# Attention in a fused kernel: the product with v streams the probabilities past the v of two heads, and a second product turns it back

## The chip, the core and the metric

The kernel runs on one core of one Trainium2 chip. The metric is device time in microseconds, of which lower is better. TensorE does matrix products (PE in the profile; the loads of its stationary operand are listed as PEld), VectorE is DVE, ScalarE ACT, GpSimd POOL, and SyncE (SP) starts most transfers.

## The reference

Attention for 4 batches of 8 heads of 576 rows, 64 wide, in which a query sees itself and the 127 keys before it; its output feeds two mixture layers, of which only the first part matters here: the gate of the first mixture takes the logits from the attention output.

```python
B, H, S, D = q.shape                                   # 4, 8, 576, 64
scores = scale * np.matmul(q, k.transpose(0, 1, 3, 2))
bias = slopes[:, None, None] * (-np.abs(rel))[None]
mask = (rel >= 0) & (rel < 128)
scores = np.where(mask, scores + bias[None], -1e9)
attn = softmax(scores)                                 # over keys
x = np.matmul(attn, v)                                 # -> (B * S, H * D) = (2304, 512)
logits = x @ w_gate                                    # 512 x 8; each row goes to the expert of its largest logit
# first mixture: x by expert, relu(x @ w1[e]) @ w2[e]; second mixture: 4 dense experts, mixed by domain_probs
```

## The kernel before

Everything is float32 or the pair of float32r values (high and low part) that stand for one. The first 190 us or so are attention; after that come the sparse mixture and, over the last two thirds, the dense one, which the change does not touch.

**Tiling.** A head has QT = 5 query tiles of 128, 128, 128, 128 and 64 rows. Tile 0 sees one block of 128 keys, the others two (the last one 128 and 64). A pair is two heads, and there are NP = 16 pairs, four a batch. A step is one tile of one head, and a duo is two steps, so that there are 80 duos, five for each pair. Steps are counted through a head before the next one, so that the five duos of a pair are tiles (0,1), (2,3), (4,0), (1,2), (3,4).

**Order.** Each engine runs one loop over duo numbers, written out in the program. TensorE in round j does `scores(j)` (L1570, L1571: q times the high and the low part of k, two float32r products a step), one tile of `gate_v` (L1613), `turn_probs(j-2)` (L1582, transposes of the probabilities against an identity), and `pv(j-4)` (L1599). VectorE adds mask and position bias and takes the maximum (`mask_scores`, L1144), ScalarE exponentiates (`soften`, L862) and copies the transposed probabilities out of PSUM (`copy_turned`, L870).

**The product with v.** `pv` has the turned probabilities stationary (128 keys x 128 queries) and streams v of one head. v has 73 useful columns a head: 64 of v, a column of ones whose product is the softmax denominator, and 8 columns v x w_gate, which `gate_v` computes ahead from a transposed copy of v (`v_turned`, loaded by SyncE) and ScalarE copies into place (`copy_vg`, L876). The stream is made 102 columns wide (PV_N), that of `gate_v` 86 (VG_N). A float32 product is listed as two passes, each with its load of the stationary operand. When a head's five tiles are done, VectorE takes denominators, reciprocals and two products out of PSUM (`norm_sum`, `norm_inverse`, `norm`; L1156, L1160, L1165, L1167), once a head.

**What else the rounds carry.** While pair n runs, the q and k of pair n+1 are split: VectorE casts (`split_hi`, L1106, two in each of the first two rounds of a pair) and GpSimd subtracts (`split_qk`, L569 and L577). TensorE's `scores` waits for it at the pair's start (`qk_lo`). When a batch's last head is done, its routing runs on VectorE a step a round: `batch_due(j, after)` says in which round, counted from round 20 + PV_LAG of the batch. Step 8 is `add_ranks` (L1270), step 9 `put`, after which GpSimd scatters the rows of x to their experts (`scatter`, L618). GpSimd's own order is fixed: for batch 0 the scatter stands between `split_qk(7)` and `split_qk(8)`, and for batch 1 the choice of the first experts (`chosen`, step 15, L1298), weight loads and a scatter stand ahead of `split_qk(13)`. After the loop GpSimd scatters batch 2, upon which SyncE loads the first rows (L494) and TensorE turns them in round 82 (`turn_rows(0)`, L1631), ahead of the `pv` of the last duo.

## Time and profile before

| | us |
|---|---|
| median of 3 runs | 1217.76 (1215.81 to 1221.4) |
| the profiled execution's own time | 1216.41 |
| its span, first to last instruction | 1214.8 |
| TensorE busy in the span | 1192.8 (98%) |
| VectorE, ScalarE, GpSimd busy | 726.4, 420.0, 794.2 |
| mean granted TensorE clock | 0.996 |
| loads of v with ones; of v turned | 16 x 365.0 KB; 16 x 288.0 KB |

Busy is the union of an engine's instructions; a TensorE product's listed duration is longer than the distance to the next one, because products overlap. What a product costs in a stream is therefore read from the distance between starts. A granted clock of 1.00 is 2.4 GHz, and 0.50 is 1.2 GHz.

### The profile page before, as it was taken

How to read it: one execution, taken by the hardware profiler on the slowest of the kernel's cores; microseconds unless marked ns; L12 is line 12 of the kernel's file. 1: busy time of each engine (PE TensorE's matmuls, PEld its weight loads, DVE VectorE, ACT ScalarE, POOL GpSimd, SP SyncE). 2: the span in 40 equal slices, each digit the busy share in tenths (PEclk: the TensorE clock that was granted, in tenths of full speed). 3: DMA queues.
4: the chain of work that ended last, by engine and by line, in shares of the span. 5: the costliest groups of instructions: out<-in, count | busy, mean ns of one | idle time of the engine just before them, and what ended most of it. 6: DMA issues, size and time to landing. Idle time of an engine off the chain costs nothing.

```text
span 1214.8 us, 18910 instructions
## 1 busy us (share of the span) xinstructions
PE 1192.8 (98%) x6446; PEld 1051.0 (87%) x6447; DVE 726.4 (60%) x1600; ACT 420.0 (35%) x766; POOL 794.2 (65%) x527
## 2 busy tenths in 40 slices
PE   8999999999999999999999999999999999999997
PEld 6888887788888888999889999999999999899996
DVE  7876987232222247666666666666666666666664
ACT  5655552111111143333333333333333333333330
POOL 5465685856666766658758776678578676666652
PEclk9998999999999999999999999999999999999999
DMA  7855687988888703212111132121211221111101
GB/s 280 278 199 175 244 310 242 338 308 320 320 319 320 304 27 123 79 53 77 70 70 70 70 122 96 70 87 62 86 70 70 81 92 60 66 68 70 70 35 52
DMA packets 46635, 177.79 MB, mean 146 GB/s; under 512 B 9312, under 2 KB 15584, under 8 KB 30176
## 3 DMA queue, kind: packets, MB, share of 16 engines
q1 hardware_dynamic: 29680, 121.57, 28.0%
q0 software_dynamic: 7520, 43.07, 9.6%
q10 hardware_dynamic: 9360, 12.17, 3.0%
q8 instruction: 45, 0.74, 0.2%
q14 instruction: 30, 0.25, 0.1%
HBM read 157.51 MB, written 19.36 MB: 146 GB/s over the span
## 4 chain that ended last, share of the span: by engine, by line
PE 91%; DVE 3%; POOL 2%; DMA 1%; issue 1%; POOLq 0%; ACT 0%; ACTq 0%; SPq 0%; DVEq 0%
PE ps L1835 33%; PE ps L1778 29%; PE ps L1692 9%; PE ps L1676 9%; PE ps L1599 4%; PE ps L1582 2%; PE ps L1703 1%; PE ps L1570 1%; DVE qk_split L1106 1%; PE ps L1571 1%; PE ps L1613 1%; PE ps L1631 1%; DVE scores_probs L1144 1%; POOL k_lo L569 1%; DMA x_rows<-x_by_expert 1%
## 5 line engine op out<-in xcount | busy, mean ns | idle before, releaser
L1525 DVE SCALAR_TENSOR_TENSOR out_sums<-ps,share_token,out_sums 128x512 f32<-128x512 f32 x270 | 202.4, 750 | 134.5 <-PE ps L1835 133.3
L1835 PE MATMUL ps<-w_hi,h_hi 128*128 128x512 f32 x576 | 226.7, 394 | 0.0
L1835 PE MATMUL ps<-w_hi,h_lo 128*128 128x512 f32 x576 | 226.3, 393 | 0.0
L1778 PE MATMUL ps<-x_hi,w_hi 128*128 128x384 f32 x672 | 224.8, 334 | 1.2 <-DVE h_lo L1509 1.2
L1835 PE MATMUL ps<-w_lo,h_hi 128*128 128x512 f32 x576 | 225.9, 392 | 0.0
L1778 PE MATMUL ps<-x_lo,w_hi 128*128 128x384 f32 x672 | 224.8, 335 | 0.0
L1778 PE MATMUL ps<-x_hi,w_lo 128*128 128x384 f32 x672 | 224.8, 334 | 0.0
L751 POOL TENSOR_TENSOR w_lo<-w_raw,w_hi 128x1024 fp32r<-128x1024 f32 x48 | 115.3, 2403 | 160.6 <-ACT w_hi L1012 160.5
L629 POOL TENSOR_TENSOR w_split<-w_raw,w_split 128x2048 fp32r<-128x2048 f32 x31 | 142.4, 4600 | 63.4 <-DMA w_split<-weights 41.2
L1039 ACT ACTIVATE h_hi<-ps 128x384 fp32r<-128x384 f32 x192 | 90.4, 493 | 206.3 <-DVE ps L1494 152.1
L746 POOL TENSOR_TENSOR w_lo<-w_raw,w_hi 128x1024 fp32r<-128x1024 f32 x48 | 115.9, 2415 | 55.1 <-ACT w_hi L1023 55.0
L727 POOL TENSOR_TENSOR w_raw<-w_raw 128x256 f32<-128x256 f32 x188 | 138.8, 738 | 14.8
L1012 ACT CAST w_hi<-w_raw 128x1024 fp32r<-128x1024 f32 x47 | 49.6, 1055 | 264.6 <-PE ps L1835 264.6
L1778 PEld LDWEIGHTS ps<-x_hi,w_hi 128*128 128x128 f32 x672 | 126.2, 188 | 3.5 <-issue 1.5
L1835 PEld LDWEIGHTS ps<-w_hi,h_lo 128*128 128x128 f32 x576 | 108.2, 188 | 24.1
L1778 PEld LDWEIGHTS ps<-x_hi,w_lo 128*128 128x128 f32 x672 | 126.2, 188 | 2.0
L1835 PEld LDWEIGHTS ps<-w_lo,h_hi 128*128 128x128 f32 x576 | 108.4, 188 | 22.3
L1835 PEld LDWEIGHTS ps<-w_hi,h_hi 128*128 128x128 f32 x576 | 108.4, 188 | 22.3
L1778 PEld LDWEIGHTS ps<-x_lo,w_hi 128*128 128x128 f32 x672 | 126.1, 188 | 0.0
L1509 DVE SCALAR_TENSOR_TENSOR h_lo<-ps,h_hi 128x384 fp32r<-128x384 f32 x192 | 106.0, 552 | 12.6 <-ACT h_hi L1039 7.5
L1676 PE MATMUL ps<-w_split,x_t_hi 128*128 (+1 forms) x336 | 105.6, 395 | 2.1 <-DVE x_t_lo L1176 1.7
L1692 PE MATMUL ps<-w_split,h_t_hi 128*128 (+1 forms) x320 | 100.9, 396 | 0.7 <-DVE y L1197 0.7
(229 smaller groups left out, 1912.4 us busy)
## 6 DMA issues: line engine op xcount, KB each, us to landing
w_raw<-weights SPq DMA_DIRECT2D x80, 1024.0 KB, 4.8
w_split<-weights POOLq DMA_DIRECT2D x32, 1024.0 KB, 8.6
qk_raw<-q_k_turned SPq DMA_DIRECT2D x16, 1152.0 KB, 6.8
v_one<-v_ones SPq DMA_DIRECT2D x16, 365.0 KB, 3.4
y_sorted<-y ACTq DMA_DIRECT2D x20, 256.0 KB, 2.6
x_rows<-x_by_expert ACTq DMA_DIRECT2D x19, 256.0 KB, 4.2
v_t<-v_turned SPq DMA_DIRECT2D x16, 288.0 KB, 7.2
x_by_expert<-zeros SPq DMA_DIRECT2D x16, 260.0 KB, 7.4
```

The lines of the kernel that those rows point to most:

```text
L629: g.tensor_tensor(Wl[slot][:, c, :], raw[:, i % 2, :], Wh[slot][:, c, :].bitcast(F32), ALU.subtract).then_inc(split_done, 1)
L727: g.tensor_tensor(to, x, y, op).then_inc(w_sums, 1)
L746: g.tensor_tensor(Ul[u % 2][:, 3:7].rearrange("p o x -> p (o x)"), raw[:, sums_at(u), 0:4 * KC * P], Uh[u % 2][:, 3:7].rearrange("p o x -> ...
L751: g.tensor_tensor(W2l[u % 2][:].rearrange("p f x -> p (f x)"), raw[:, u % 2, 4 * KC * P:UNIT], W2h[u % 2][:].rearrange("p f x -> p (f x)") ...
L1012: a.copy(W2h[u % 2][:].rearrange("p f x -> p (f x)"), raw[:, u % 2, 4 * KC * P:UNIT]).then_inc(w2_hi, 1)
L1039: a.activation(Hh[u % 2][:, f, half * HALF_T:(half + 1) * HALF_T], ps[:, bank, 0:HALF_T], ACT.Relu).then_inc(h2_hi, 1)
L1509: v.scalar_tensor_tensor(out=Hl[u % 2][:, f, cols], in0=ps[:, bank, 0:HALF_T], scalar=0.0, in1=Hh[u % 2][:, f, cols].bitcast(F32), op0=ALU ...
L1525: v.scalar_tensor_tensor(out=a_, in0=ps[:, 4 + t % 3, :], scalar=share_, in1=a_, op0=ALU.mult, op1=ALU.add).then_inc(acc_done, 1)
L1676: last = mm(ps[:, half, :], x[:, c, :], part(w, half, c * HALF), start=(k == 0), stop=(k == 3 * DC - 1))
L1692: last = mm(ps[:, y_bank(i), :], h[:, f, :], part(w, 2 + half, f % n * D), start=(f == 0 and k == 0), stop=(f == 2 * n - 1 and k == 2))
L1778: last = mm(ps[:, bank, 0:HALF_T], wt[:, w, c * P:(c + 1) * P], xt[:, c, x, :], start=(k == 0), stop=(k == 3 * KC - 1))
L1835: last = mm(ps[:, 4 + t % 3, :], ht[:, f, t * P:(t + 1) * P], wt[:, f, :], start=(k == 0), stop=(k == n - 1))
```

## The change

`pv` is turned round. Now v is stationary (keys x 64 columns of one head), and the turned probabilities stream, 128 columns wide. The two heads of a pair write different halves of the PSUM partitions, 0 to 63 and 64 to 127. A duo is now one tile of both heads of a pair, and `scores`, `mask_scores`, `soften`, `turn_probs` are regrouped accordingly (both heads' last tiles, of 64 rows, fall into one duo). The result has the output's columns on partitions, so VectorE copies it to SBUF (`copy_heads`, one a duo) and a second product (`back`, one a duo) multiplies it by an identity with 16 gate columns beside it, 144 columns wide: that turns it back and gives the two heads' gate logits. `gate_v`, `copy_vg`, the column of ones and the loads of `v_turned` go. The denominator comes from ScalarE's exponential (`accum_out`), summed and inverted once a pair (`sum_den`, `turn_den`). `norm` runs twice a pair, for tiles 0 to 2 and 3 to 4. The loops are one round longer, and `batch_due` counts from one round later (BACK_LAG for PV_LAG). GpSimd copies the identity four times at the start.

```diff
-VB = DH + 1 + E1
-V_COLS = QT * 2 * VB
-PV_N = 102
-VG_N = 86
+V_COLS = QT * 2 * DH
+BACK = P + 2 * E1
+LOW_TILES = 3
...
         PV_LAG = 4
-        LAGS = PV_LAG + 1
-        VG_LEAD = 4
+        BACK_LAG = PV_LAG + 1
+        LAGS = BACK_LAG + 1
...
         def batch_due(j, after):
-            at = j - (QT * PAIRS + PV_LAG) - after
+            at = j - (QT * PAIRS + BACK_LAG) - after
...
             load_qk(0, 0)
-            load_vt(0, 0)
-            sp.dma_start(wg_sb[:], w_gate).then_inc(gate_in, 16)
             load_qk(1, 1)
-            load_vt(1, 1)
             load_v(0, 0)
+            sp.dma_start(wb_sb[:, :, P:BACK], w_gate.rearrange("p (n e) -> p n e", n=PAIRS)).then_inc(gate_in, 16)
             load_v(1, 1)
-            sp.wait_ge(vg_done, 1)
-            load_vt(2, 0)
...
-                sp.wait_ge(heads_normed, n * 2)
+                sp.wait_ge(pv_done, (n - 1) * QT)
                 load_v(n, n % 2)
...
+            g.tensor_copy(wb_sb[:, :, 0:P], ident[:].unsqueeze(1).broadcast_to([P, PAIRS, P])).then_inc(back_ident, 1)
...
             def soften(j):
-                for s in (2 * j, 2 * j + 1):
-                    w, m, slot = window(s % QT)[1], ROWS[s % QT], s % (2 * SOFT_DUOS)
+                n, t = divmod(j, QT)
+                w, m = window(t)[1], ROWS[t]
+                if t == 0 and n >= 2:
+                    act.wait_ge(den_summed, n - 1)
+                for hd in range(2):
+                    s = 2 * j + hd
+                    slot = s % (2 * SOFT_DUOS)
                     act.wait_ge(scores_masked, s + 1 + 2 * BANKS)
                     ins = a.activation(sp_sb[0:m, slot, 0:w], sp_sb[0:m, slot, 0:w], ACT.Exp,
-                                       bias=low[0:m, slot:slot + 1], scale=-1.0)
+                                       bias=low[0:m, slot:slot + 1], scale=-1.0,
+                                       accum_out=den[0:m, n % 2, t, hd, 0:1])
                 ins.then_inc(probs_ready, 1)
...
+            def copy_heads(j):
+                m, at = ROWS[j % QT], j % OT_BUFFERS
+                if j >= OT_BUFFERS:
+                    dve.wait_ge(back_done, j - OT_BUFFERS + 1)
+                dve.wait_ge(pv_done, j + 1)
+                v.tensor_copy(ot_sb[:, at, 0:m], ps[:, 4 + j % BANKS, 0:m]).then_inc(heads_copied, 1)
+            def sum_den(n):
+                dve.wait_ge(probs_ready, n * QT + QT)
+                if n > 0:
+                    dve.wait_ge(den_turned, n)
+                v.tensor_reduce(den_sum[:], den[:, n % 2], AX.X, ALU.add).then_inc(den_summed, 1)
+            def turn_den(n):
+                dve.wait_ge(den_summed, n + 1)
+                dve.wait_ge(heads_normed, 2 * n)
+                v.reciprocal(rden[:, n % 2], den_sum[:]).then_inc(den_turned, 1)
+            def norm(n, part):
+                first, end = ((0, LOW_TILES), (LOW_TILES, QT))[part]
+                nt = end - first
+                b, p = divmod(n, PAIRS)
+                dve.wait_ge(den_turned, n + 1)
+                dve.wait_ge(back_done, n * QT + end)
+                x = ps[:, 6 + part, 0:nt * BACK].rearrange("p (t e) -> p t e", e=BACK)
+                d = rden[:, n % 2, first:end]
+                v.tensor_tensor(lg_sb[:, 2 * p:2 * p + 2, first:end].rearrange("p h t e -> p t h e"),
+                                x[:, :, P:BACK].rearrange("p t (h e) -> p t h e", h=2),
+                                d.unsqueeze(3).broadcast_to([P, nt, 2, E1]), ALU.mult)
+                v.tensor_tensor(x_sb[:, b * QT + first:b * QT + end, p * P:(p + 1) * P]
+                                .rearrange("p t (h e) -> p t h e", h=2),
+                                x[:, :, 0:P].rearrange("p t (h e) -> p t h e", h=2),
+                                d.unsqueeze(3).broadcast_to([P, nt, 2, DH]), ALU.mult).then_inc(heads_normed, 1)
+            def sum_six(n):
+                dve.wait_ge(heads_normed, 2 + 2 * n + 2)
+                link(v.tensor_reduce(part_l[:], lg_sb[:, 0:H - 2].rearrange("p h t e -> p t e h"), AX.X, ALU.add))
...
             for j in range(DUOS + LAGS):
-                heads = head_due(j)
-                for h in heads:
-                    norm_sum(h)
                 if j < DUOS:
                     mask_scores(2 * j)
                 for b in batch_due(j, 6):
                     read_ranks(b)
-                for h in heads:
-                    norm_inverse(h)
                 if j < DUOS:
                     mask_scores(2 * j + 1)
-                for h in heads:
-                    norm(h)
-                    if h % H == H - 2:
-                        sum_seven(h)
+                if 0 <= j - PV_LAG < DUOS:
+                    copy_heads(j - PV_LAG)
+                for n in pair_due(j, QT + 1):
+                    sum_den(n)
+                    turn_den(n)
+                for n in pair_due(j, BACK_LAG + LOW_TILES):
+                    norm(n, 0)
+                for n in pair_due(j, BACK_LAG + QT):
+                    norm(n, 1)
+                    if n % PAIRS == PAIRS - 2:
+                        sum_six(n)
                 if 1 <= j // QT < NP - 1:
                     for a_, h_ in SPLIT_AT[j % QT]:
                         split_hi(j // QT + 1, a_, h_)
...
                 for b in batch_due(j, 0):
                     sum_logits(b)
...
             def pv(j):
                 pe.wait_ge(turned_copied, j + 1 + BANKS)
-                c0 = 0
-                for s in (2 * j, 2 * j + 1):
-                    h, t = s // QT, s % QT
-                    m = ROWS[t]
-                    if t == 0:
-                        pe.wait_ge(heads_normed, h + 1)
-                        if h % 2 == 0:
-                            pe.wait_ge(vg_copied, h // 2 + 1)
-                    blocks = key_blocks(t)
-                    for i, (kb, _, w) in enumerate(blocks):
-                        v0 = (kb * 2 + h % 2) * VB
-                        last = mm(ps[0:m, 4 + h % 2, t * PV_N:(t + 1) * PV_N],
-                                  pt_sb[0:w, j % SOFT_DUOS, c0 + i * m:c0 + (i + 1) * m],
-                                  v_sb[0:w, h // 2 % 2, v0:v0 + PV_N], start=(i == 0), stop=(i == len(blocks) - 1))
-                    c0 += turned_width(t)
+                n, t = divmod(j, QT)
+                m = ROWS[t]
+                if t == 0:
+                    pe.wait_ge(v_loaded[n % 2], (n // 2 + 1) * 16)
+                if j >= BANKS:
+                    pe.wait_ge(heads_copied, j - BANKS + 1)
+                blocks = key_blocks(t)
+                for i, (kb, _, w) in enumerate(blocks):
+                    for hd in range(2):
+                        c0, v0 = hd * turned_width(t) + i * m, (kb * 2 + hd) * DH
+                        last = mm(ps[hd * DH:(hd + 1) * DH, 4 + j % BANKS, 0:m], v_sb[0:w, n % 2, v0:v0 + DH],
+                                  pt_sb[0:w, j % SOFT_DUOS, c0:c0 + m], start=(i == 0), stop=(i == len(blocks) - 1))
                 last.then_inc(pv_done, 1)
-            def gate_v(n, t):
-                k = n % 2
-                if t == 0:
-                    pe.wait_ge(vt_in[k], (n // 2 + 1) * 16)
-                    if n >= 2:
-                        pe.wait_ge(vg_copied, n - 1)
-                    if n % PAIRS == 3 and n > PAIRS:
-                        pe.wait_ge(ranks_read, n // PAIRS)
-                ins = mm(ps[0:ROWS[t], 6 + k, t * VG_N:(t + 1) * VG_N], vt_sb[:, k, t * P:t * P + ROWS[t]],
-                         wg_sb[:, n % PAIRS * 2 * E1:n % PAIRS * 2 * E1 + VG_N], start=True, stop=True)
-                if t == QT - 1:
-                    ins.then_inc(vg_done, 1)
+            def back(j):
+                n, t = divmod(j, QT)
+                m = ROWS[t]
+                part, at = divmod(t, LOW_TILES)
+                if at == 0:
+                    pe.wait_ge(heads_normed, 2 * n + 1 + part)
+                if n == 0:
+                    pe.wait_ge(gate_in, 16)
+                    pe.wait_ge(back_ident, 1)
+                if part == 1 and n % PAIRS == 1 and n > PAIRS:
+                    pe.wait_ge(ranks_read, n // PAIRS)
+                pe.wait_ge(heads_copied, j + 1)
+                mm(ps[0:m, 6 + part, at * BACK:(at + 1) * BACK], ot_sb[:, j % OT_BUFFERS, 0:m],
+                   wb_sb[:, n % PAIRS, :], start=True, stop=True).then_inc(back_done, 1)
...
             for k in range(WARM_FIRST):
                 mm(ps[:, 0, 0:2 * P], ident[:], mask[:], start=True, stop=True)
-            pe.wait_ge(gate_in, 16)
-            pe.wait_ge(banks_cleared, 1)
-            for t in range(QT):
-                gate_v(0, t)
             for j in range(DUOS + LAGS):
                 if j < DUOS:
                     scores(j)
-                n, t = divmod(j + VG_LEAD, QT)
-                if 1 <= n < NP:
-                    gate_v(n, t)
                 if 0 <= j - 2 < DUOS:
                     turn_probs(j - 2)
                 if 0 <= j - PV_LAG < DUOS:
                     pv(j - PV_LAG)
+                if 0 <= j - BACK_LAG < DUOS:
+                    back(j - BACK_LAG)
```

TensorE, middle of the attention, before: one round (names as in the lines above; the shapes are stationary columns x streamed columns).

```order
L1570 MATMUL ps<-qk_split 128x256 [waits scores_masked]
L1571 MATMUL ps<-k_lo,qk_split 128x256
L1570 MATMUL ps<-qk_split 128x256
L1571 MATMUL ps<-k_lo,qk_split 128x256
L1613 MATMUL ps<-w_gate,v_t 128x86
L1582 MATMUL ps<-ident,scores_probs 128x128 [waits turned_copied,probs_ready]
L1582 MATMUL ps<-ident,scores_probs 128x128 x3
L1599 MATMUL ps<-v_one,probs_t 128x102 [waits turned_copied]
```

TensorE, the same place, after.

```order
L1578 MATMUL ps<-qk_split 128x256 [waits scores_masked]
L1579 MATMUL ps<-k_lo,qk_split 128x256
L1590 MATMUL ps<-ident,scores_probs 128x64 [waits turned_copied,probs_ready]
L1590 MATMUL ps<-ident,scores_probs 64x64
L1590 MATMUL ps<-ident,scores_probs 128x64
L1590 MATMUL ps<-ident,scores_probs 64x64
L1606 MATMUL ps<-probs_t,v 64x128 [waits heads_copied,turned_copied]
L1606 MATMUL ps<-probs_t,v 64x128 x3
L1622 MATMUL ps<-ident_gate,heads_t 128x144 [waits heads_copied]
```

The product before `pv` is gone, `pv` has 64 stationary columns in every duo instead of 128, waits for the copy of two duos ago, and a product of 144 columns stands behind it.

VectorE, the second round of a pair, after (`heads_t` is what `copy_heads` writes).

```order
L1134 ISA scores_probs,neg_max<-ps,alibi 128x256 [waits scores_ready]
L1134 ISA neg_max 128x1
L1134 ISA scores_probs,neg_max<-ps,alibi 128x256
L1134 ISA neg_max 128x1
L1146 COPY heads_t<-ps 128x128 [waits pv_done,back_done]
L1153 TENSOR_REDUCE den_sum<-den 128x10 [waits den_turned,probs_ready]
L1158 RECIPROCAL rden<-den_sum 128x10 [waits heads_normed,den_summed]
L1094 CAST qk_split<-qk_raw 128x576 [waits qk_in1] x2
```

Before, the casts stood right behind the masking; now the copy stands between them, and it waits for the `pv` that ends the same round on TensorE.

## Rows read from the trace of the kernel before

**Rows 1.** The profile page, its head and its first part.
```profile
span 1214.8 us, 18910 instructions
PE 1192.8 (98%) x6446; PEld 1051.0 (87%) x6447; DVE 726.4 (60%) x1600; ACT 420.0 (35%) x766; POOL 794.2 (65%) x527
```

**Rows 2.** Windows of pairs 2, 5, 7, 12, 14; busy, clock, DMA share, GB/s.
```profile
27.05:37.49 10.44, 10.44 (x87) 9.11 (x86) 7.61 (x33) 7.02 (x19) 5.28 (x2) 1.00 0.84 277
...
58.37:69.27 10.90, 10.90 (x92) 9.57 (x90) 9.72 (x42) 6.16 (x18) 5.34 (x2) 1.00 0.52 191
...
79.71:91.78 12.07, 10.66 (x87) 9.17 (x86) 7.44 (x39) 7.64 (x20) 8.54 (x5) 1.00 0.72 228
...
137.03:148.56 11.53, 10.67 (x87) 9.18 (x85) 10.40 (x51) 7.44 (x19) 7.88 (x5) 1.00 0.74 260
...
159.47:171.63 12.16, 10.92 (x86) 9.27 (x86) 11.38 (x33) 4.97 (x15) 9.90 (x5) 1.00 0.91 366
```

**Rows 3.** The chain of waits, 38 to 48.5 us, about one pair.
```profile
by line: PE ps L1599 44.5%; PE ps L1582 21.0%; PE ps L1570 14.4%; PE ps L1613 10.6%; PE ps L1571 10.5%
...
39.07 0.87 PE ps L1599 x8
...
44.62 0.44 PE ps L1582 x4
45.06 1.06 PE ps L1599 x8
```

**Rows 4.** Timeline of TensorE, stretches of 80.1 to 88.8 us: start, duration.
```profile
80.13 0.28 PE L1571 MATMUL ps<-k_lo,qk_split 128*128 128x256 f32 x1
80.34 0.36 PE L1613 MATMUL ps<-w_gate,v_t 128*64 128x86 f32 x2
80.63 0.33 PE L1582 MATMUL ps<-ident,scores_probs 128*128 128x128 f32 x1
...
87.64 0.30 PE L1599 MATMUL ps<-v_one,probs_t 128*64 128x102 f32 x1
...
88.27 0.38 PE L1570 MATMUL ps<-qk_split 128*128 128x256 f32 x1
88.49 0.28 PE L1571 MATMUL ps<-k_lo,qk_split 128*128 128x256 f32 x1
88.61 0.25 PE L1570 MATMUL ps<-qk_split 128*64 128x192 f32 x1
```

**Rows 5.** Groups of VectorE and ScalarE, 27 to 80 us: busy, mean ns.
```profile
L1167 DVE TENSOR_TENSOR x<-ps,rden 128x320 f32<-128x320 f32 x10 | 4.7, 472 | 0.0
...
L1156 DVE TENSOR_SCALAR den<-ps 128x5 f32<-128x5 f32 x10 | 1.6, 160 | 1.1 <-PE ps L1599 0.9
...
L1260 DVE COPY ranks_counts<-ps 128x80 f32<-128x80 f32 x1 | 0.2, 238 | 0.0
...
L876 ACT COPY v_one<-ps 128x80 f32<-128x80 f32 x5 | 1.1, 225 | 0.0
```

**Rows 6.** The chain of waits, from stretches 74 to 92 and 133 to 150 us.
```profile
76.67 1.30 DVE token_row L1270
...
78.17 4.30 issue
...
137.56 0.17 DVE first_experts L1298
```

**Rows 7.** A window in which the granted clock was 0.50.
```profile
91.75:98.57 6.82, 6.79 (x30) 5.80 (x30) 2.86 (x12) 2.42 (x6) 4.50 (x3) 0.50 0.92 292
```

**Rows 8.** Line L494 (issue and landing of the first rows), and timeline.
```profile
L494 SPq DMA_DIRECT2D x_rows<-x_by_expert x2: 333/368/403, 181.7 to 183.1; - x2
...
DMA to landing us min/median/max: 2.6/2.7/2.8
...
185.16 0.60 PE L1631 MATMUL ps<-ident,x_rows 128*128 128x128 f32 x4
```

**Rows 9.** The chain of waits at the start of the program.
```profile
1.40 0.42 SPq L444
```

132 lines of the change are left out of this document (52 added, 80 removed).

## Prediction

> **What bounds the kernel now.** The page's first part says that TensorE is busy 98% of the span [rows 1], but that is a mean over three stages, of which only the attention is changed. So I cut the attention into its pairs of heads, by the starts of each pair's first score product, and looked at the windows [rows 2]. In an undisturbed pair TensorE is busy for all of its 10.44 us and VectorE for 7.6 of them; eleven of the sixteen pairs take 10.4 or, with a batch's two rank products, 10.9 us. There TensorE's own work sets the pace. Three later pairs are longer (12.07, 11.53, 12.16 us), TensorE has idle time in them, and in the last two of them VectorE is busy 10.4 and 11.4 us: there VectorE and GpSimd set it. I therefore need two things: what the new products cost on TensorE, and whether VectorE and the chains behind the three long pairs leave room for a gain.
>
> The chain of waits over one pair [rows 3] divides the pair on TensorE: of 10.5 us, 44.5% or 4.67 us is `pv`, 21% or 2.2 us the transposes, 10.6% or 1.1 us `gate_v`, the rest, 2.6 us, the scores. Eight passes of `pv` with 128 stationary columns take 0.87 us, 0.109 a pass, whatever is listed as one's duration. Four transposes, which stream 128 columns each, take 0.44 us: so a float32 pass of 128 streamed columns costs 0.109 too, and I take the stream as 0.109 x columns / 128 (102 columns: 0.087). The 102-column stream is thus shorter than its pass; the load of 128 stationary columns sets that.
>
> The timeline shows what 64 stationary columns cost in float32 [rows 4]. The gate product with 64 of them starts 0.21 us after the score product ahead of it, where such score products follow each other by 0.11 to 0.12: 0.09 of pause on entry. Its two passes take 0.29 us until the next product starts, against 2 x 0.073 for their streams: 0.05 for a load that nothing hides, 0.09 of pause on leaving. Four `pv` passes, two with 128 x 64 and two with 64 x 64, take 0.63 us (87.64 to 88.27), which is 4 x 0.087 + 2 x (0.05 + 0.09). And the first product of 128 columns behind them takes 0.22 instead of 0.11: its load is uncovered as well. The float32r scores with 64 columns (88.61, 0.12 behind the one before) show no pause. So the array changes shape for float32 with 64 columns, and a visit costs 0.09 + 0.05 on the way in and 0.09 + 0.11 on the way out, 0.34 us.
>
> **The change on TensorE, for one pair.** Today only the two 64-row tiles pay such visits. After it every `pv` does, since v has 64 columns a head. The open price is the stream: whether passes of two heads, in two halves of the array, run at once. The trace of before never uses the second half, so I bound it. One after the other, a duo's eight passes of 128 columns cost 0.87 us. At once, the order a1 a2 b1 b2 a3 a4 b3 b4 (two passes a head, passes of one head can't overlap) leaves five slots, 0.55 us. A full halving would be 0.44.
>
> Tiles 1 to 3: 0.87 + 0.34 = 1.21 or 0.55 + 0.34 = 0.89, against 0.87. Tile 0: four passes, 0.44 + 0.34 = 0.78 or 0.33 + 0.34 = 0.67. The last tile: eight passes of 64 columns in two shapes, 8 x 0.055 + 0.48 = 0.92 or 6 x 0.055 + 0.48 = 0.81. Sum of `pv`: 5.33 or 4.15, against 4.67 now. `back` is two passes of 144 columns, 0.245, five times 1.23, for the 1.1 of `gate_v`. The transposes keep their number, but both 64-row tiles now share one visit: 1.9 for 2.2. Scores no longer stand behind a 64-column `pv`: about 2.25 for 2.45 (of the rest of 2.6, the window being 10.5). Together **10.7 us one after the other, 9.5 at once**, against 10.44.
>
> I take "at once". The halves have their own stationary columns and their own PSUM partitions, and the rows show that a load of 0.19 us already runs beside a stream. The Trainium skill says the same of the halves (TensorEngine Tiling (Array Packing), Key Properties: different tiles execute loads and products in parallel); no row here shows that for the streams. There is a rule of it against the change: in TensorE: Matmul & The Clock Gate, Part 3, a load overlaps products in flight only when its row group differs, and two heads side by side share theirs. By that rule each of 36 passes would show its load of 0.05 and the pair would cost 12.5 us; for one shape [rows 3] contradict it, with passes at the pace of their loads and no stream added on top.
>
> **VectorE.** `copy_heads` is new, five a pair; the nearest row is the 128 x 80 copy out of PSUM, 0.24 us [rows 5], between nothing (hidden in its idle time) and that: 1.2 us. The product that writes x covers the same 640 columns a pair, 0.47 us per 320, in pieces of 384 and 256. Of the four small operations on denominators at 0.16 two remain: -0.3. So VectorE gets 0.9 us more a pair: 8.5 in pair 2, which still fits into 9.5, but 10.6 in pair 5 [rows 2]. Besides, `copy_heads` waits for the `pv` that ends the same round, and casts and norms are queued behind it; TensorE needs the copy one round later, so this costs only where VectorE is already late. ScalarE: what `accum_out` adds is in no row; between nothing and one more small operation a tile (0.22 us, the smallest row), 2.2 a pair on 7.0, less the 0.22 of `copy_vg`. It then has 9.0 of 9.5, so I take it as hidden. Transfers: 288 KB less a pair on queues that nobody in the attention waits for; at the start one issue of 0.42 us [rows 9] and that of the gate weights no longer stand ahead of the second q and k: -0.5 us, between 0 and -0.9.
>
> **The round that is added.** `batch_due` is one round later, and what hangs on it is pinned to GpSimd's order. Pair 8 starts when `split_qk(8)` is done; it stands behind the scatter of batch 0, that behind `put` (VectorE's token row at 76.67, blocked 1.3 us by a GpSimd operation; then GpSimd from 78.17 [rows 6]). One round, 2.0 us, later, less 0.7, since the subtraction that blocked it will mostly be over: +1.3. TensorE stood idle for it 1.6 us at 90 us and its granted clock then was 0.50 for 6.82 us [rows 7], which costs 3.4 us, now as before. The choice of experts (137.56) holds back pair 13 in the same way: +2.0. That stall was 0.9 us and the clock stayed; at about 3 us I expect a fall as the other: +3.4. At the end the first rows are asked for at 181.7, land 2.7 us later and are turned at 185.16 [rows 8], 0.8 us of slack: a round later TensorE waits 1.3 us, with the last `pv` queued behind it; the last duo's copy and `back` add 0.4.
>
> **The sum**, against the profiled execution's own time, 1216.4: start -0.5; pairs 1 to 6: three with room at -0.9, the others limited by VectorE at -0.5 together, -3.2; pair 8 +1.3; pairs 8 to 11 -0.9; pair 13 +2.0 and clock +3.4; pairs 13 to 15: VectorE +0.9 in pair 14 and -0.5 in pair 15; end +1.7. That is +4.2, 1220.6. The median of the runs is 1.35 above this execution: **1222 us**. What a measurement of this kernel can tell from no change is about 0.5%, 6 us.
>
> **Rivals.** (1) *One after the other*: +0.26 in the 12 pairs that do not wait, 3.1, start -0.5, +1.3, +2.0, +3.4, VectorE 0.9, end +1.7: +12, 1230. For it: nothing in the trace shows two streams at once. (2) *The other side, a gain*: VectorE's waits give way (its casts are blocked by GpSimd for different lengths, and it idles 2.8 us in pair 2), the clock does not fall a second time: 15 pairs at -0.92, less 3 for pairs that wait, +1.3 and +1.7 for the round: -8, 1209. It decides if the pairs 4 to 11 run at 9.5 to 9.8. (3) *Loads or changes of head uncovered*: 0.05 a pass is 1.8 us a pair on top of 10.7, +2.1 x 15: 1250. (4) *The clock*: half the array idles in `pv`. Each fall as in rows 7 costs 3.4 us; five of them beyond my sum are 1239. Against it: the streams cover more of a round than today.
>
> **How the numbers follow.** Forecast 0.42 (1216 to 1228), rival 1 0.27 (1225 to 1236), rival 2 0.18 (1202 to 1212), rival 3 0.07, rival 4 0.06. The range 1208 to 1237 leaves out the lower part of rival 2 and most of 3 and 4, some 0.18. Faster by over 0.5% (below 1211.7) is rival 2: 0.18. Within: three quarters of the forecast and a little of rival 1: 0.37. Slower (above 1223.8): 0.45.
>
> **What would show it.** Right, if pairs 2 and 3 take about 9.5 us with starts of `pv` passes in five slots of 0.11; 10.7 and eight equal distances mean rival 1. A pause must stand on both sides of every `pv`, with 0.05 and 0.11 of load. VectorE must be busy 0.9 us more a pair, and pairs 4 and 5 stay near 10.4. Pair 8 and pair 13 must start a round later relative to their neighbours, with clock 0.50 behind both. The prediction is wrong if ScalarE's accumulation makes it late (a wait of TensorE's transposes for the probabilities), if the clock stays low longer, or if the added round is absorbed.

## The result and the profile after

The changed kernel takes **1245.71 us** (median of 4 runs, 1245.27 to 1250.64), the kernel before on the same chip 1217.97: the ratio is 1.0237, with a 95% interval of 1.0222 to 1.0253. It is slower by 28 us; forecast were 1222 and a range of 1208 to 1237. The profiled execution took 1245.62 us. The head of its page:

```profile
span 1243.6 us, 19316 instructions
PE 1192.2 (96%) x6446; PEld 1034.8 (83%) x6447; DVE 743.4 (60%) x1653; ACT 430.3 (35%) x910; POOL 795.0 (64%) x527
PEclk9997789999999999999999999999999999999999
```

TensorE is busy as long as before [rows 1], yet the span is 28.8 us longer: its work did not grow, its idle time and its slow time did. The windows of pairs 2, 3, 4, 5, 6, 7, 8, 10 and 14, cut as in [rows 2] (busy us of PE, PEld, DVE, ACT, POOL, then the granted clock):

```profile
27.00:37.05 10.05, 9.36 (x86) 7.30 (x85) 9.10 (x41) 7.22 (x28) 5.29 (x2) 1.00 0.75 242
37.05:46.85 9.80, 9.19 (x86) 7.24 (x85) 8.62 (x34) 6.77 (x26) 5.29 (x2) 1.00 0.85 263
46.85:58.29 11.44, 9.27 (x85) 7.24 (x84) 10.70 (x51) 6.86 (x26) 5.28 (x2) 1.00 0.76 228
58.29:69.62 11.33, 9.40 (x85) 7.21 (x85) 10.08 (x37) 6.47 (x25) 5.39 (x2) 1.00 0.47 148
69.62:81.35 11.73, 10.01 (x89) 7.75 (x88) 10.62 (x44) 7.03 (x27) 5.51 (x3) 1.00 0.36 127
81.35:95.56 14.21, 9.26 (x85) 7.28 (x85) 8.56 (x46) 8.94 (x33) 8.36 (x5) 1.00 0.42 156
95.56:109.01 13.45, 13.45 (x84) 10.73 (x85) 8.79 (x36) 6.15 (x23) 7.17 (x4) 0.62 0.41 127
120.63:135.87 15.24, 15.04 (x89) 12.01 (x88) 9.75 (x46) 7.40 (x27) 5.48 (x3) 0.59 0.19 72
173.40:191.19 17.79, 13.31 (x90) 10.45 (x89) 14.24 (x48) 7.66 (x29) 10.73 (x6) 0.71 0.55 199
```

TensorE's own pair has fallen from 10.44 to 9.2 to 9.4 us, as wanted. But only pairs 2 and 3 are clearly shorter than before. In pairs 4 to 6 VectorE is busy 10.1 to 10.7 us, more than TensorE, and the pair is longer than either. From pair 8 on the clock is also down for long stretches. What TensorE and VectorE wait for, from 20 to 215 us (total us, times, longest):

```profile
POOL k_lo L558 <- DVE qk_split L1094: 48.9, 11, 6.7
...
PE ps L1622 <- DVE heads_t L1146: 20.3, 17, 3.9
DVE heads_t L1146 <- PE ps L1606: 18.9, 26, 1.7
```

`back` waits for VectorE's copy, and VectorE's copy waits for `pv`: a two-way wait that the kernel before did not have. The timeline of VectorE, GpSimd and TensorE shows one such round in pair 4 (start, us, and in brackets the idle time ahead and what ended it):

```profile
51.93 2.64 POOL L558 TENSOR_TENSOR k_lo<-qk_raw,qk_split 128x1152 fp32r<-128x1152 f32 x1 [5.33 <-DVE qk_split L1094]
...
52.92 2.34 DVE L1094 CAST qk_split<-qk_raw 128x576 fp32r<-128x576 f32 x2
...
54.41 0.60 PE L1606 MATMUL ps<-probs_t,v 128*64 128x64 f32 x8
...
55.18 0.41 DVE L1134 CUSTOM_DVE_ANT_0 scores_probs<-ps,alibi 128x256 f32<-128x256 f32 x1
...
55.87 0.28 DVE L1146 COPY heads_t<-ps 128x128 f32<-128x128 f32 x1
...
56.29 0.36 PE L1622 MATMUL ps<-ident_gate,heads_t 128*128 128x144 f32 x1 [1.29 <-DVE heads_t L1146]
```

GpSimd's subtraction of k runs from 51.93 to 54.57. Of the two casts behind it on VectorE the first starts under it and takes 1.97 us; the two take 2.34 us together, where two that start beside nothing take 0.9. Behind them in VectorE's queue stand two masks and then the copy, which ends at 56.1, and TensorE has been idle since 55.0. The result of the old `pv` was read by VectorE's norms twice in five rounds (once a head); the new one needs VectorE in each round.

The half clock, in two of its five windows (the others start at 146.70 and 177.40 for 10.24 us and at 201.30 for 3.40 us; there is one of 3.4 us at the start too):

```profile
95.50:105.74 10.24, 10.18 (x53) 8.16 (x54) 6.61 (x24) 3.75 (x15) 5.82 (x4) 0.50 0.48 154
119.40:133.05 13.65, 12.89 (x63) 10.14 (x64) 8.57 (x42) 6.96 (x25) 5.48 (x3) 0.50 0.24 88
```

That is 48 us at half clock where the kernel before had 6.8 [rows 7]. Each begins in or up to 1.4 us behind idle time of TensorE of 1.6 to 4.9 us in one or two pieces. Idle times of 1.01 and 0.79 us in pair 5 were followed by none.

The longest pair, 14, has its own cause. The chain of waits there:

```profile
173.07 0.47 DVE x L1172
173.53 4.62 DVE onehot L1254
...
178.94 0.20 DVE heads_t L1146
```

One small routing step of 40 columns (`onehot`) takes 4.70 us on VectorE, while GpSimd subtracts a weight tile from 173.56 to 178.08 us (`w_split`, L619). The same step takes 0.19 us for batches 0 and 1, and 1.33 us at this place in the kernel before, where it was over before GpSimd's operation began. The copy stands behind it, `back` waits 3.9 us, and 10.24 us at half clock follow.

**Where the 28.8 us of the two profiled executions lie**, by the starts of the pairs: pair 0 and the start -0.3 us; pairs 1 to 6 +1.9 (63.1 to 65.0); pair 7 +2.1; pairs 8 to 11 +7.0 (45.3 to 52.2); pairs 12 to 14 +8.8 (34.6 to 43.4); from pair 15 to the first expert product +4.5 (which starts at 211.32 for 187.28); behind it +4.8.

### The profile page after: what moved, and what is told of

The parts are those of the page before. It is cut to its first block, busy times and chain, and to the rows that moved or that the text cites. A ratio compares the mean times of both kernels' runs of the same rounds, so it can differ in the third digit from the quotient of the medians.

```text
span 1243.6 us, 19316 instructions
## 1 busy us (share of the span) xinstructions
PE 1192.2 (96%) x6446; PEld 1034.8 (83%) x6447; DVE 743.4 (60%) x1653; ACT 430.3 (35%) x910; POOL 795.0 (64%) x527
## 4 chain that ended last, share of the span: by engine, by line
PE 88%; DVE 6%; DMA 2%; issue 2%; POOL 1%; ACT 1%; ACTq 0%; POOLq 0%; DVEq 0%
PE ps L1836 32%; PE ps L1779 28%; PE ps L1693 9%; PE ps L1677 8%; PE ps L1606 3%; PE ps L1590 2%; DMA x_rows<-x_by_expert 2%; PE ps L1622 2%; PE ps L1704 1%; DVE qk_split L1094 1%; PE ps L1578 1%; DVE scores_probs L1134 1%; PE ps L1579 1%; PE ps L1638 1%; DVE heads_t L1146 0%
## 5 line engine op out<-in xcount | busy, mean ns | idle before, releaser
L619 POOL TENSOR_TENSOR w_split<-w_raw,w_split 128x2048 fp32r<-128x2048 f32 x31 | 142.3, 4596 | 66.4 <-DMA w_split<-weights 42.8
L1519 DVE SCALAR_TENSOR_TENSOR h_lo<-ps,h_hi 128x384 fp32r<-128x384 f32 x192 | 106.2, 553 | 12.3 <-ACT h_hi L1027 7.2
L859 ACT ACTIVATE scores_probs<-scores_probs,neg_max 128x256 f32<-128x256 f32 (+2 forms) x160 | 74.9, 469 | 83.3 <-DVE neg_max L1134 80.3
```

The source lines that it names most:

```text
L619: g.tensor_tensor(Wl[slot][:, c, :], raw[:, i % 2, :], Wh[slot][:, c, :].bitcast(F32), ALU.subtract).then_inc(split_done, 1)
L859: ins = a.activation(sp_sb[0:m, slot, 0:w], sp_sb[0:m, slot, 0:w], ACT.Exp, bias=low[0:m, slot:slot + 1], scale=-1.0, accum_out=den[0:m, n ...
L1519: v.scalar_tensor_tensor(out=Hl[u % 2][:, f, cols], in0=ps[:, bank, 0:HALF_T], scalar=0.0, in1=Hh[u % 2][:, f, cols].bitcast(F32), op0=ALU ...
```

## Experiments

**1 and 2. The added round and VectorE's added copy, each put into the kernel before.**

```
-            at = j - (QT * PAIRS + PV_LAG) - after
+            at = j - (QT * PAIRS + PV_LAG + 1) - after
```

> The kernel before, with one number changed: everything that hangs on batch_due (sum of the logits, choice, ranks, scatter) comes one round later, as in the changed kernel; the attention product is the old one. Theory A (VectorE's queue): the added round is a small part; by the prediction's own terms +1.3 for pair 8, +2.0 for pair 13, at most +3.4 for a second fall of the clock, +1.3 at the end, so 1220 to 1226 us. Rival C (the added round is the cause, since routing and GpSimd's order are pinned to it): 1235 or more, with the half clock at several places.

Measured: 1224.94 us, ratio 1.0083 (1.0065 to 1.0101), +10 us. The terms of the forecast for the round (1.3, 2.0, 3.4 and 1.3) make 8.0: the sum holds. Of the terms only the first does: pair 7 is 13.50 us long, 1.43 more than before, for 1.3. Pair 12, which was to bring 2.0, brings 0.75; pairs 13 and 14 bring 1.2 and 3.5, with half clock behind; and the stretch from pair 15 to the first expert product, which was to bring 1.3, brings none.

The second run adds to this, between the two masks of a duo:

```
+                    v.tensor_copy(idle_copy[0:ROWS[j % QT], j % 4, :], ps[0:ROWS[j % QT], j % BANKS, 0:P])
```

> The kernel before with routing one round later, as the run that gave 1.008, and in each round one more copy of 128 x 128 out of PSUM on VectorE between the two mask products, into a buffer that nobody reads. It prices VectorE's added work without a consumer and under the old, slower product of TensorE. If the work alone makes the loss: 1232 or more. Theory A (what costs is that TensorE waits for this copy a round later, and that the pair is now shorter than VectorE's and GpSimd's chain): within 4 us of the run with the late round alone, so 1223 to 1230.

Measured: 1228.47 us, ratio 1.0109 (1.0080 to 1.0139). Its windows of pairs 4 and 5:

```profile
48.01:58.45 10.44, 10.44 (x86) 9.12 (x86) 10.34 (x45) 6.64 (x16) 5.28 (x2) 1.00 0.74 243
58.45:68.90 10.45, 10.45 (x87) 9.12 (x86) 9.58 (x41) 6.33 (x18) 5.35 (x2) 1.00 0.60 217
```

VectorE is busy 10.34 us of 10.44 and TensorE waits for nothing. A copy that nobody waits for costs 3 us under the old product, with intervals that overlap; nearly the same VectorE time in the changed kernel goes with pairs of 11.3 to 11.7.

**3 to 6. The copy and the casts moved.** Run 3 has `copy_heads` on ScalarE:

```
-                if 0 <= j - PV_LAG < DUOS:          (VectorE)
-                    copy_heads(j - PV_LAG)
+                if 0 <= j - BACK_LAG < DUOS:        (ScalarE, behind copy_turned)
+                    copy_heads(j - BACK_LAG)
```

> The changed kernel, with the copy of the transposed heads on ScalarE (35% busy) in place of VectorE, between its copy of the turned probabilities and the exponentials. Theory A (back and pv wait for a copy that stands in VectorE's queue behind casts which GpSimd blocks): the waits of back for heads_t, 20 us, go, pairs 4 to 6 fall from 11.4 to below 10, the clock falls less often, and the time is 1215 to 1228 us. Rival B (ScalarE with its accumulator reads is late as well): the waits move to ScalarE, 1240 or more. Rival D (the clock falls because of what pv does to the array, not because of waits): pairs shorten but the half clock stays at some 40 us or more, 1232 to 1240.

Measured: 1235.87 us, ratio 1.0156 (1.0128 to 1.0184). It gives back a third of the loss, but not as theory A said: `back` still waits 17.1 us for the copy, now ScalarE's, whose queue waits for the masks. Pairs 4 and 5 take 11.0 and 11.6. The half clock before the experts stays at 55 us, and the time lies in the range of rival D, that `pv` itself pulls the clock down; runs 16 and 17 speak against that.

Run 4 has all casts ahead of GpSimd's subtractions:

```
-                    for a_, h_ in SPLIT_AT[j % QT]:
+                    for a_, h_ in (PIECES if j % QT == 0 else []):
-                    pool.wait_ge(qk_hi, (p - 2) * 4 + 2)
+                    pool.wait_ge(qk_hi, (p - 2) * 4 + 4)
```

> The changed kernel, with the four casts of a pair all in its first round and GpSimd's subtractions waiting for all four, so that no cast is queued on VectorE while GpSimd works on the same pair's k. Theory A: casts take 0.45 us each and not 1.7 to 2.5, the copy comes in time, pairs 4 to 6 fall to 9.5 to 10.3, 1222 to 1234 us in all (routing steps stay blocked by GpSimd). If VectorE is late by its own work alone (0.9 us more a pair) and not by the block: no change, 1243 to 1248. GpSimd starts 1 us earlier or later by pair; a wait for its split at the starts of the pairs would show that it has become the bound.

Measured: 1239.52 us, ratio 1.0177 (1.0135 to 1.0219). Every cast now takes 0.45 us and pairs 1 to 3 take 9.30, 9.64 and 9.65; pairs 4 to 6 stay at 11.2 to 11.5, and the time lies between the two ranges. Its chain of waits, from pair 4 on:

```profile
50.09 0.83 DVE qk_split L1094 x2
51.06 2.66 POOL k_lo L558
53.79 2.65 POOL qk_split L566
56.44 0.14 issue
56.57 0.30 PE ps L1578
...
64.35 1.83 DVE token_row L1249
```

Once VectorE reaches the casts late, GpSimd's 5.3 us behind them no longer fit into the pair and hold up the next one's scores; and the routing steps are blocked in place of the casts (`token_row`, 1.83 us for 40 columns).

Run 5 has both edits.

> The changed kernel with both edits of before: the copy of the heads on ScalarE, and the four casts in a pair's first round with GpSimd waiting for all four. Each alone took back a third to a quarter of the loss and left pairs 4 to 6 at 11 to 11.6 us. Theory A (VectorE's queue and GpSimd's blocks bound the pairs together): pairs 1 to 6 at 9.3 to 10, the sum of the two gains or more, 1220 to 1231. Rival G (what is left is the chain casts, then 2 x 2.65 us of GpSimd, then the next pair's scores, which the two edits do not shorten): pairs 4 to 6 stay near 11, 1230 to 1238.

Measured: 1244.41 us, ratio 1.0215 (1.0198 to 1.0232): the gains do not add, and the expectation missed. Pairs 1 to 3 are short, 9.44, 8.97 and 8.96 us, but then pair 4, behind the setup for routing on VectorE (`share`), takes 14.05 with the clock at half for 6.8 us, and six more such stretches of 6.8 to 13.7 us follow before the experts.

Run 6 takes VectorE's work away without touching the copy: q's two casts go to ScalarE.

```
+                if 1 <= j // QT < NP - 1 and j % QT == 1:      (ScalarE)
+                    for a_, h_ in PIECES[2:4]:
+                        cast_q(j // QT + 1, a_, h_)
-                    for a_, h_ in SPLIT_AT[j % QT]:            (VectorE)
+                    for a_, h_ in (PIECES[0:2] if j % QT == 0 else []):
```

> The changed kernel with the two casts of q of each pair on ScalarE, in the pair's second round, and the two of k on VectorE in its first; no cast is left on VectorE while GpSimd subtracts, and VectorE has 0.9 us less a pair. Theory A: back's waits for its copy go, except in the rounds with routing steps, 1225 to 1236. If ScalarE's in-order queue is then late (its casts are 0.7 us each ahead of the copy of the turned probabilities): waits of pv for probs_t, and 1240 or more.

Measured: 1232.80 us, ratio 1.0133 (1.0117 to 1.0150), the best single edit: 12 to 13 us back. It takes away both 0.9 us of VectorE's work a pair and the casts that GpSimd holds up. Its windows of pairs 2, 4, 5 and 7, and waits from 20 to 205 us:

```profile
25.42:34.65 9.23, 9.16 (x86) 7.24 (x85) 6.65 (x34) 7.83 (x29) 5.30 (x2) 1.00 0.92 274
43.88:54.59 10.71, 9.23 (x86) 7.22 (x85) 8.45 (x48) 8.27 (x29) 5.30 (x2) 1.00 0.79 245
54.59:65.27 10.68, 9.35 (x85) 7.20 (x84) 9.43 (x35) 7.22 (x26) 5.34 (x2) 1.00 0.54 168
76.83:93.22 16.39, 9.38 (x86) 7.30 (x85) 8.11 (x44) 9.92 (x35) 8.34 (x5) 0.87 0.38 135
```

```profile
DVE heads_t L1155 <- PE ps L1615: 19.9, 34, 1.9
...
PE ps L1631 <- DVE heads_t L1155: 11.8, 9, 3.9
```

Pair 2 is bound by TensorE at last (9.16 of 9.23 us). Pairs 4 and 5 still take 10.7, with both engines busy less than 9.5: there `back` waits 0.7 and 0.9 us for the copy and the transposes 0.8 and 0.4 us for ScalarE. In pair 14, 18.19 us long, `onehot` takes 4.69 us again and `back` waits 3.9.

**7. The two heads one after the other.**

```
-                for i, (kb, _, w) in enumerate(blocks):
-                    for hd in range(2):
+                for hd in range(2):
+                    for i, (kb, _, w) in enumerate(blocks):
```

> The changed kernel with pv's loops exchanged: all key blocks of one head, then all of the other, so that no two neighbouring products lie in different halves of the array. The trace of the changed kernel shows a full duo's pv at 0.59 us with a start of both heads 7 ns apart. If the gain of pv comes from this overlap: pv about 1.0 to 1.05 us a duo (8 x 0.109 and the two edges), TensorE's work 11.0 to 11.4 a pair in place of 9.35. Theory A (VectorE and GpSimd set 4 of 5 pairs): most of those 1.8 us are hidden in the long pairs, the idle time falls, the clock falls less, and the time is 1240 to 1256. If TensorE sets the time: 15 x 1.8 more, 1268 to 1275.

Measured: 1248.66 us, ratio 1.0248 (1.0226 to 1.0270), the same as the changed kernel. But the run did not do what it was made for. The timeline of a full duo, in the changed kernel and then in this one:

```profile
31.91 0.66 PE L1606 MATMUL ps<-probs_t,v 128*64 128x128 f32 x8
```

```profile
30.76 0.66 PE L1606 MATMUL ps<-probs_t,v 128*64 128x128 f32 x8
```

Eight passes in 0.66 us in both, where eight at the old distance are 0.87: the heads run side by side even when all of one is issued ahead of the other. So this run can't say what the overlap is worth; run 9 prices TensorE's pace.

**8 to 10. Which engine's time counts.** Run 8 makes VectorE's copy twice:

```
+                v.tensor_copy(idle_copy[:, at, 0:m], ps[:, 4 + j % BANKS, 0:m])
                 v.tensor_copy(ot_sb[:, at, 0:m], ps[:, 4 + j % BANKS, 0:m]).then_inc(heads_copied, 1)
```

> The changed kernel with VectorE's copy of the heads made twice, the first into a buffer that nobody reads: 0.20 us more a round, 1.0 a pair, on VectorE, with the wait and its place in the queue as they are. If VectorE's amount of work bounds the pairs from the fourth on: +1.0 for each of 12 pairs and the lengths of pairs 1 to 3 nearly as before, +10 to +16, 1255 to 1262. If the order and the waits bound them, and VectorE has room: +0 to +4, 1243 to 1250.

Measured: 1258.07 us, ratio 1.0335 (1.0300 to 1.0370), 12 us more than the changed kernel for 1.0 us of VectorE a pair. The run does not separate VectorE's amount of work from the wait: the idle copy stands ahead of the one that `back` waits for, and so lengthens that wait too. Pairs 1 to 3 are 0.1 to 0.3 us longer, pairs 4 and 5 0.6 each (12.01 and 11.95), and pair 6 3.8 (15.53, at a mean clock of 0.60). With 72 us of half clock before the experts for 51, part of the 12 us is clock.

Run 9 makes TensorE's pair 1.1 us longer, by a product without a use in each round (`back` ahead of its wait):

```
+                    mm(ps[:, 6 + part, 432 - part * 80:512 - part * 80], ident[:], mask[:, 0:80], start=True, stop=True)
```

> The changed kernel with one product of 128 x 80 whose result is not used in every round ahead of back's wait: 0.22 us a round, 1.1 a pair, so that TensorE's own pair is back at 10.4. If the gain on TensorE is not cashed in from the fourth pair on: only pairs 1 to 3 get longer, 1243 to 1249, perhaps less, since the clock has more activity. If TensorE's pace matters everywhere: +15 us, 1258 to 1262.

Measured: 1247.35 us, ratio 1.0238 (1.0220 to 1.0255), the changed kernel's to 0.01%. Its windows of pairs 2, 4, 5, 6 and 10, beside the ones above:

```profile
27.36:38.07 10.71, 10.56 (x95) 8.45 (x94) 9.34 (x41) 7.89 (x31) 5.28 (x2) 1.00 0.74 233
48.45:59.84 11.39, 10.85 (x95) 8.48 (x94) 10.44 (x48) 7.24 (x28) 5.28 (x2) 1.00 0.74 228
59.84:71.16 11.32, 10.73 (x95) 8.48 (x94) 9.83 (x36) 6.04 (x23) 5.38 (x2) 1.00 0.50 148
71.16:82.88 11.72, 11.25 (x99) 8.95 (x99) 10.60 (x44) 7.03 (x27) 5.49 (x3) 1.00 0.36 129
120.35:132.06 11.71, 11.24 (x100) 8.95 (x99) 10.60 (x43) 7.00 (x27) 5.52 (x3) 1.00 0.36 128
```

Pairs 4, 5 and 6 keep their lengths (11.44, 11.33, 11.73 without the filler) with 1.2 to 1.6 us more of TensorE in them. Pairs 7 and 13, also at full clock in both, take 14.22 and 11.34 for 14.21 and 11.33. Among these pairs only 2 and 3 pay, so the gain of the new product on TensorE is worth nothing in the others. That the totals agree is partly luck: the filler also cut the half clock before the experts from 51 to 27 us, so that pairs 8 and 10 are 1.5 and 3.5 us shorter, while pairs 11 and 14 are 2.6 and 1.1 longer.

Run 10 gives the two-way wait one more round:

```
-        BACK_LAG = PV_LAG + 1
+        BACK_LAG = PV_LAG + 2
```

> The changed kernel with back one more round behind pv (and the routing one more round late with it). TensorE then needs a copy two rounds after its pv, in back as in the reuse of pv's bank, so VectorE may be late by one round more. If the tight two-way wait is the cause: pairs 4 to 6 at 10.7 or less (VectorE's busy time), the waits of back for heads_t (26 us before) under 8, 1228 to 1238 in spite of the later routing. If VectorE's work and GpSimd's blocks are the cause: pairs 4 to 6 stay at 11.3 to 11.7 and the time is 1243 to 1252.

Measured: 1238.77 us, ratio 1.0185 (1.0142 to 1.0229). Pairs 4 and 5 take 10.84 and 9.96 us, pair 6 12.93 (mean clock 0.87):

```profile
47.33:58.17 10.84, 9.43 (x86) 7.25 (x86) 9.52 (x51) 6.86 (x26) 5.28 (x2) 1.00 0.78 241
58.17:68.13 9.96, 9.40 (x86) 7.27 (x86) 9.10 (x35) 5.81 (x22) 5.33 (x2) 1.00 0.47 153
```

VectorE is busy 9.5 and 9.1 us in them for 10.7 and 10.1, with the same instructions in pair 4: the cast that GpSimd holds up takes 0.84 us for 1.97 there. So VectorE's busy time is not only its work; some of it depends on when the casts come. TensorE's waits, from 20 to 215 us, beside those of the changed kernel:

```profile
PE ps L1578 <- POOL qk_split L566: 12.2, 3, 6.4
PE ps L1590 <- ACT probs_t L868: 9.5, 14, 2.7
PE ps L1629 <- DVE x L1172: 5.9, 3, 4.2
```

The 20.3 us of waits for `heads_t` are gone, 12.2 us for GpSimd's split have come (4.9 before the edit), and 9.5 for ScalarE's turned probabilities (0.3). GpSimd's scatters wait 11.3 us for the places from VectorE, for 7.3: the routing is a round later still.

**11. Both reliefs.** Run 6's edit with `BACK_LAG = PV_LAG + 2`.

> q's casts on ScalarE (alone 1.0133) together with back one more round behind pv. If both VectorE's load and the tight wait count: pairs 4 to 6 at 9.5 to 10.2 and 1218 to 1228. If the late routing takes it back, pairs 7 and 14 stay at 16 to 18 and the time is 1230 to 1238.

Measured: 1240.09 us, ratio 1.0165 (1.0125 to 1.0206), pairs 1 to 4 at 8.8 to 9.95, but pairs 5 and 6 at 12.3 and 11.2, and pairs 7, 12 and 14 at 15.8, 16.2 and 16.8: the second half of the expectation, 2 us above its range.

**12. The copy at the start of the next round.** VectorE's own waits of 18.9 us for `pv` were the suspect.

> The changed kernel with VectorE's copy of a duo's heads at the start of the next round, ahead of the masks, in place of behind the masks of its own round. In the changed kernel VectorE itself waits 18.9 us, in 26 rounds, for the pv of the same round before it can go on to the casts and norms behind the copy. Theory V (this wait of VectorE is what makes its queue late: TensorE waits for VectorE, then VectorE for TensorE): 1226 to 1236, pairs 4 to 6 below 10.8. Theory A in its first form (only the blocked casts count): the copy now stands behind the same casts, nothing gained, 1242 to 1250.

Measured: 1245.64 us, ratio 1.0227 (1.0210 to 1.0244). Nothing gained: theory V falls. VectorE waits less for `pv` (6.3 us) but TensorE more for the copy (28.4 us for 20.3).

**13. ScalarE without its accumulation** (`accum_out` left out).

> The changed kernel without the accumulation of the exponentials' sums on ScalarE; the denominators are then left at 1, so x and the logits are not divided by the sums (the token routing differs). It takes ten register reads of 0.18 us a pair off ScalarE. Rival B (ScalarE's longer chain from the mask to the probabilities delays TensorE): 1232 to 1240. If it is hidden, as the prediction had it: within 3 us of the changed kernel, apart from what other routing does to the last stage.

Measured: 1275.84 us, ratio 1.0487 (1.0463 to 1.0512), with other routing in the last stage, so that only the attention can be read: the first expert product starts at 209.2 us in place of 211.3. The accumulation is nearly hidden; rival B falls.

**14 and 15. The added round taken out of the changed kernel**: the rank products go to the gate bank that is free a round sooner, and the steps behind them follow.

```
-                mm(ps[:, 7, RANKS_AT:RANKS_AT + n], upper[:], oh, start=True, stop=True)
+                mm(ps[:, k, RANKS_AT:RANKS_AT + n], upper[:], oh, start=True, stop=True)
-            ROUTE = {1: shift, 2: pick, 3: mark, 4: gate_sum, 5: gate_share, 7: count, 8: add_ranks, 9: put}
+            ROUTE = {1: shift, 2: pick, 3: mark, 4: gate_sum, 5: gate_share, 6: count, 7: add_ranks, 8: put}
```

> The changed kernel with the added round taken out of the routing: the rank products go to the other gate bank, so that they need only the first three tiles of the next pair and come one round sooner; their copy, the counts, the places and the choice of experts follow one round sooner, as before the change. In the kernel before the late round alone cost 8 to 10 us. If its cost is of its own (additive): 1234 to 1238, with pair 7 nearer 12.5. If what holds up GpSimd's scatter and the choice is VectorE's lateness anyway: within 3 us of the changed kernel, 1240 to 1246.

Measured: 1245.70 us, ratio 1.0214 (1.0193 to 1.0236; one of its four times, 3275.9 us, is left out of the ratio, and nothing here explains it). The round that cost 10 us under the old product gives at most 3 here. In pair 13, now 18.5 us long, the rank product waits instead for `onehot`, which takes 4.68 us there:

```profile
PE ps L1630 <- DVE onehot L1255: 4.9, 1, 4.9
```

> The casts of q on ScalarE (alone 1.0133) together with the routing one round sooner. If the two costs are separate, VectorE's queue and the added round: 1.013 less 0.007, 1222 to 1228. If they are one cost seen twice: no better than 1.011, 1230. Faster than the kernel before needs both of them gone and the half clock under 10 us, below 1212.

Measured, with q's casts on ScalarE too: 1230.72 us, ratio 1.0130 (1.0094 to 1.0166), no better than the casts alone.

**16 and 17. The clock.** Filler products ahead of `back`'s wait, only in rounds in which TensorE was idle.

```
+        FILL_AT = {39: 20, 48: 4, 49: 3, 58: 8, 62: 3, 68: 3, 69: 3, 70: 16, 77: 3, 78: 6}
```

> The changed kernel, with products of 128 x 80 into unused columns of the gate banks in ten rounds, ahead of back's wait for its copy, where the trace shows TensorE idle for 0.8 to 4.8 us (69 products of about 0.22 us: 20 at pair 8, 16 at pair 14). They compute nothing that is used and shorten no wait. Theory T (the half clock after the stalls costs 17 to 19 us of the 28): the half clock falls from 51 us to under 15 and the time to 1228 to 1235. If the clock is a companion and not a cost (TensorE has slack while VectorE is late): the clock is up and the time stays at 1243 to 1250. If it is pv that pulls the clock down: the clock falls anyway.

Measured: 1238.91 us, ratio 1.0200 (1.0172 to 1.0228), less by 0.4% than the changed kernel, with intervals that overlap. Half clock before the experts, with the start: 20 us for 51. Its windows of pairs 10 and 13:

```profile
119.77:131.50 11.73, 10.02 (x90) 7.77 (x89) 10.61 (x44) 7.04 (x27) 5.51 (x3) 1.00 0.37 126
...
156.78:171.75 14.97, 14.97 (x97) 12.00 (x97) 11.00 (x38) 7.10 (x27) 8.69 (x5) 0.67 0.47 172
```

Pair 10, which has no filler, takes 11.73 us at full clock and 15.24 at 0.59: 3.5 us for a fall of 13.65 us. Pair 8 takes 11.68 (mean clock 0.87) for 13.45 (0.62). But one fall came back in pair 13 (11.33 before). With `pv` unchanged the clock stays at 1.00 in most pairs, so it is not `pv` alone that pulls it down.

> The kernel with q's casts on ScalarE and the rank products one round sooner (1.0130), with products whose result is not used (55 of 0.22 us) ahead of back in four rounds where its trace shows waits of 2.4, 2.4, 5.8 and 2.6 us, each followed by 6.8 to 13.7 us of half clock. If the half clock is a cost of its own: the half clock falls from 31 us to under 10 and the time by 4 to 10 us, 1220 to 1227. If it only accompanies waits that VectorE makes: within 3 us, 1228 to 1234.

Measured: 1227.69 us, ratio 1.0082 (1.0068 to 1.0097), with 10 us of half clock before the experts for 41 in run 15 (both with the start): 3 us less by the medians, 6 by the ratios. It is the best of the changed kernels, and still 10 us slower than before.

**18. The best edit in the kernel before**: q's casts on ScalarE there.

> The kernel before with the two casts of q of each pair on ScalarE in the pair's second round, the same edit that gave the changed kernel 12.6 us back. If VectorE bounds only the changed kernel: the eleven pairs of 10.4 to 10.9 us stay, the three long ones (12.07, 11.53, 12.16) lose up to 1 us each, 1213 to 1219. If VectorE's relief pays of itself: 1205 to 1211. If ScalarE's queue then delays the probabilities: 1219 or more.

Measured: 1214.70 us over 12 runs, ratio 0.9978 (0.9962 to 0.9994). The ten pairs of 10.4 to 10.9 stay, pairs 7, 12 and 14 become 11.81, 10.45 and 11.27 us. It is the only version below both kernels, by 0.2%, less than what counts as a difference here. The same edit gave 12 to 13 us in the changed kernel: VectorE's relief pays where TensorE waits for VectorE.

## Why the prediction was wrong

**Right: TensorE's share.** "I take 'at once'" holds, and more: a full duo's passes take four slots, not five, with edges of 0.17 us (0.61 us in the chain of waits less 4 x 0.109); most of the rest of the 0.34 a visit falls to `back` behind it. TensorE's pair is 9.2 to 9.4 us, and 8.96 in the shortest pair of run 5, for 9.5. The rule of the Trainium skill that different tiles run loads and products in parallel agrees (TensorEngine Tiling (Array Packing), Key Properties). The Trainium skill's rule against it (TensorE: Matmul & The Clock Gate, Part 3), by which each pass would show its load, does not: the pair would be 12.5 us.

**Right as a sum: the added round** by itself, 8.0 forecast and 10 measured. Three of its four terms came at other places or in other sizes (run 1), so that the agreement is partly luck. ScalarE's accumulation is hidden, as forecast.

**Wrong: the step on VectorE.** The text said "TensorE needs the copy one round later, so this costs only where VectorE is already late", and let pairs 4 and 5 stay near 10.4. Its amount was right: VectorE is busy 1.0 us a pair more over pairs 1 to 6, for 0.9. The wait was not. VectorE and TensorE now wait for each other within one round, and pairs 4 to 6 take 11.3 to 11.7 us with neither engine busy more than 10.7. Run 2 has nearly the same VectorE load, held-up casts and all, under the old product, and its pairs 4 and 5 stay at 10.44 and 10.45: there only masks of two rounds ago, and norms twice in five rounds, stand between VectorE and TensorE. Run 10 gives one round of slack, and pairs 4 and 5 go to 10.8 and 10.0. Run 6 takes work and held-up casts off VectorE and gives back 12 to 13 us; run 9 makes TensorE's pair 1.1 us longer, and pairs 4 to 7 do not change. Being late is no exception either: `back` waits for the copy in 17 rounds. Pairs 1 to 11, forecast at -2.8 with pair 8's start, came to +11.

The prediction also read too few pairs. It counted eleven of 10.4 to 10.9 us, where there are ten: pair 8 takes 13.48, with the half clock. It forecast -0.9 over pairs 8 to 11, though VectorE was busy 10.22 us in pair 11 before, which with its own 0.9 makes 11.1; that pair took 11.93.

**Wrong: the late pairs.** From pair 12 on the forecast had +7.5 (2.0, 3.4, 0.9, -0.5 and 1.7); measured were +18.1. The "VectorE +0.9 in pair 14" became +5.6, the half clock that followed included: `onehot` was late enough to fall under GpSimd's subtraction of 4.5 us. It does so in every variant of the changed kernel here and takes 3.9 to 4.8 us in each, against 0.2 to 1.9 in the variants of the kernel before.

**Wrong: the clock.** One fall more was forecast, and as rival 4 "five of them beyond my sum". There were five in all in the pairs, with 48 us of half clock for 6.8. The price of 3.4 us was meant for 6.8 us of half clock; pair 10 pays 3.5 us for a fall of 13.65, so that the falls are longer than forecast and cheaper for their length. Each begins in or behind idle time of TensorE of 1.6 to 4.9 us, and with TensorE otherwise behind VectorE only part of its price shows. Runs 16 and 17 put that at 3 to 7 us of the 28.

**Not additive.** By the runs the round is worth 10 us and VectorE's copy under the old product 3. The rest, about 15, exists only with the new order and its two-way wait; TensorE's shorter pair does not bring it, since run 9 makes the pair long again and the loss stays. The round costs 10 alone and gives 3 when taken out: each late chain (VectorE's queue, GpSimd's split behind it, the routing) hides the others. The best changed kernel (run 17) gets back some 18 of the 28 us; no run here gets back the other 10.

**Open.** The regrouping of the duos came with the new product and was never run by itself; what it adds to the lateness is not shown. The 4.8 us behind the first expert product were not tested. In the trace the chain waits there twice for rows of x, from 229.93 us for 4.32 and from 235.66 for 9.35, where the kernel before waits once, from 211.28 for 7.89; that they are late because the scatters are is only argued. The 6.56 us of "issue" ahead of the scatter in pair 7, for the 4.30 of [rows 6], are mostly the late routing: the places are ready 3.2 us after GpSimd is free, 1.2 before the change. The remaining 3.4 and 3.1 us are unexplained.
